# Routing on VectorE in two places: owners behind the state, running counts in front of the masking

## What is computed

```python
def _attn_ref(r, k, v, w, u):
    for t in range(S):
        kt, vt, rt = (k[:, :, t], v[:, :, t], r[:, :, t])
        cur = np.einsum('bhd,bhe->bhde', u[None] * kt, vt)
        y[:, :, t] = np.einsum('bhd,bhde->bhe', rt, state + cur)
        state = w[None, :, :, None] * state + np.einsum('bhd,bhe->bhde', kt, vt)

def _moe_ref(x, w_gate, w1, w2, capacity):
    logits = x @ w_gate
    expert_idx = np.argmax(logits, axis=1)
    ...
    for i in range(N):
        e = expert_idx[i]
        if counts[e] < capacity:
            disp[e, counts[e]] = x[i]
            pos[i] = counts[e]
            counts[e] += 1
            keep[i] = True
    h = np.maximum(np.einsum('ecd,edf->ecf', disp, w1), 0.0)
    y = np.einsum('ecf,efd->ecd', h, w2)
    for i in range(N):
        if keep[i]:
            out[i] = gate_w[i] * y[expert_idx[i], pos[i]]

def _moe2_ref(x, w_in, w_out):
    h = x @ w_in
    g = h - np.tanh(h)
    return (g @ w_out).astype(np.float32)
```

## Time and profile before

| | us |
|---|---|
| median of 3 runs | 419.5 |
| lowest, highest | 415.28, 419.82 |
| the profiled execution | 416.17 |
| its span in the trace | 414.4 |
| TensorE busy in the span | 392.7 |
| VectorE busy | 211.5 |
| ScalarE busy | 182.5 |
| GpSimd busy | 155.2 |

### The profile page before, as it was taken

One profiled execution on the slowest core, in us unless ns is written; L12 is line 12 of the kernel. 1 busy time (PEld: TensorE's weight loads), 2 busy tenths in 40 slices (PEclk: granted clock), 3 DMA queues, 4 the chain that ended last, 5 costly groups with the idle time before them and its releaser, 6 DMA issues.

```text
span 414.4 us, 10465 instructions
## 1 busy us (share of the span) xinstructions
PE 392.7 (95%) x3736; PEld 380.8 (92%) x3737; DVE 211.5 (51%) x453; ACT 182.5 (44%) x486; POOL 155.2 (37%) x132
## 2 busy tenths in 40 slices
PE   5999898999999999999999899999999999999991
PEld 4787777989999999999999899999999999999991
DVE  6365888655556455465455556524343434334340
ACT  5354456432666656657566354533132312231220
POOL 3564676604888815427246043352001100020002
PEclk9999999558999999999999999999999999999997
DMA  7488987443678585685776725101000100010001
GB/s 249 137 253 264 270 247 215 134 153 119 202 241 253 190 269 172 229 262 175 244 232 204 229 69 182 56 1 57 0 0 3 54 0 0 0 57 0 0 1 63
DMA packets 48454, 56.85 MB, mean 137 GB/s; under 512 B 3585, under 2 KB 46017, under 8 KB 48417
## 3 DMA queue, kind: packets, MB, share of 16 engines
q1 hardware_dynamic: 35936, 46.23, 35.5%
q10 hardware_dynamic: 10512, 5.31, 4.5%
q0 software_dynamic: 1968, 4.83, 3.1%
HBM read 46.23 MB, written 10.13 MB: 136 GB/s over the span
## 4 chain that ended last, share of the span: by engine, by line
PE 89%; DVE 5%; issue 2%; DMA 1%; ACT 1%; POOL 0%; POOLq 0%; SPq 0%; DVEq 0%; ACTq 0%
PE ring L1065 13%; PE ring L1067 13%; PE ring L1066 13%; PE pO L1317 8%; PE pO L1316 8%; PE pO L1065 5%; PE pO L1067 5%; PE pO L1066 5%; PE pY L1189 3%; PE pA L1140 2%; PE pD L1094 2%; PE ring L1205 2%; PE pY L1174 1%; PE ring L1254 1%; DVE kw L784 1%
## 5 line engine op out<-in xcount | busy, mean ns | idle before, releaser
L459 POOL TENSOR_TENSOR w_lo<-raw_weights,w_hi 128x768 fp32r<-128x768 f32 x40 | 73.7, 1845 | 85.1 <-ACT w_hi L580 84.9
L1007 DVE SCALAR_TENSOR_TENSOR minus_tanh<-square,ring 128x384 f32<-128x384 f32 x64 | 35.5, 554 | 93.3 <-ACT square L730 93.3
L580 ACT ACTIVATE w_hi<-raw_weights 128x768 fp32r<-128x768 f32 x80 | 67.1, 846 | 24.3 <-DMA raw_weights<-w 24.2
L730 ACT ACTIVATE square<-ring 128x384 f32<-128x384 f32 x64 | 31.5, 491 | 94.3 <-DVE h_hi L1017 53.8
L1065 PE MATMUL ring<-yT_hi,w_hi 128*128 x192 | 65.0, 338 | 1.7 <-DVEq L1002 1.7
L1067 PE MATMUL ring<-yT_hi,w_lo 128*128 x192 | 64.9, 338 | 0.0
L1316 PE MATMUL pO<-w_hi,h_hi 128*128 128x384 f32 x192 | 64.9, 338 | 0.0
L1317 PE MATMUL pO<-w_lo,h_hi 128*128 128x384 f32 x192 | 64.8, 338 | 0.0
L1066 PE MATMUL ring<-yT_lo,w_hi 128*128 x192 | 64.8, 338 | 0.0
L1065 PE MATMUL pO<-h_hi,w_hi 128*128 128x224 f32 x192 | 53.3, 278 | 0.0
L550 POOL DMA_INDIRECT out<-out_rows,tok x12 | 11.7, 974 | 111.1 <-ACT out_rows L725 107.2
(11 more groups left out here) (158 smaller groups left out, 762.3 us busy)
## 6 DMA issues: line engine op xcount, KB each, us to landing
raw_weights<-w SPq DMA_DIRECT2D x80, 384.0 KB, 4.0
x_by_slot<-x ACTq DMA_DIRECT2D x9, 576.0 KB, 5.8
x_expert<-x_by_slot SPq DMA_DIRECT2D x8, 576.0 KB, 5.6
kv<-kv_by_token SPq DMA_DIRECT2D x22, 192.0 KB, 4.3
rkT<-rk_by_feature SPq DMA_DIRECT2D x18, 192.0 KB, 3.8
rkT<-rk_by_feature SPq DMA_DIRECT2D x3, 512.0 KB, 5.3
x_expert<-x_by_slot SPq DMA_DIRECT2D x1, 384.0 KB, 3.0
x_by_slot<-x,sloti POOLq DMA_INDIRECT x12, 4.6
```

The source lines that it names most:

```text
L459: pool.tensor_tensor(lo, unit_raw(2, k), hi.bitcast(F32), ALU.subtract).then_inc(w2_ready, 1)
L580: act.activation(hi, unit_raw(what, k), ACT.Copy).then_inc(w1_hi if what == 1 else w2_hi, 1)
L730: act.activation(sq[:, i % 2, :], ring[i % 4][:, 0:CAP], ACT.Square, scale=THIRD ** 0.5, accum_out=sqsum[:, bass.ds(t * (2 * FC) + i, 1)]) ...
L1007: dve.scalar_tensor_tensor(out=nt[:, i % 2, :], in0=sq[:, i % 2, :], scalar=1.0, in1=ring[i % 4][:, 0:CAP], op0=ALU.subtract, op1=ALU.mult ...
```

## The change

`route1` is cut in two. `owners_of` keeps the steps up to `onehot`; `counts_of` has the `upto` additions, `oh_ready` and `slot_limit`. For groups 0 and 1, `owners_of` stands where `route1` stood, at the end of iterations 5 and 9 (`OWNERS`), and `counts_of` stands in iterations 6 and 10 (`COUNTS`) behind `queries` and in front of the masking. Groups 2 and 3 run both halves one behind the other, as before. The first `low` moves from the end of iteration 10, in front of `route2(1)`, into iteration 11, behind `output(10)` and in front of the last masking. No instruction is added or taken away on any engine, and nothing moves on the others. Of what VectorE waits for, one thing is new: the `x` behind `owners_of` waits for the chain semaphore of `onehot`.

```diff
-ROUTE1 = {5: 0, 9: 1}
+OWNERS = {5: 0, 9: 1}
+COUNTS = {6: 0, 10: 1}
...
-            def route1(g, link):
+            def owners_of(g, link):
...
                 link(dve.tensor_tensor(onehot[:, 0:m], bc(prio[:, :].unsqueeze(1), [P, m, E]),
                                        bc(owners.unsqueeze(2), [P, m, E]), ALU.is_equal))
+
+            def counts_of(g, link):
+
+                first, m = GROUPS[g]
+                owners = allf[:, 0, first:first + m]
                 for i in range(m):
                     link(dve.tensor_tensor(upto[:, first + i + 1, :], upto[:, first + i, :], onehot[:, i, :], ALU.add))
                 dve.sem_inc(oh_ready, 1)
...
                 if n + 1 < STEPS:
                     queries(n + 1)
+                else:
+                    low(0, 0, 0)
+                if n in COUNTS:
+                    counts_of(COUNTS[n], rlink)
                 dve.wait_ge(a_full, n + 1)
...
-                if n == STEPS - 2:
-                    low(0, 0, 0)
                 if n == STEPS - 1:
-                    route1(2, rlink)
+                    owners_of(2, rlink)
+                    counts_of(2, rlink)
                     low(0, 1, 0)
                 if n in ROUTE2:
                     route2(ROUTE2[n], rlink)
-                if n in ROUTE1:
-                    route1(ROUTE1[n], rlink)
+                if n in OWNERS:
+                    owners_of(OWNERS[n], rlink)
...
-            route1(3, rlink)
+            owners_of(3, rlink)
+            counts_of(3, rlink)
```

## The result

The changed kernel took 425.2 us in the median of 4 runs (423.8 to 428.2), the kernel before 417.4 in 4 runs beside it (415.2 to 419.8). The ratio is 1.028, 95% interval 1.022 to 1.035; this ratio and all that follow are taken over undisturbed runs alone and can lie up to 0.9% away from the quotient of the two medians, which is 1.019 here. The profiled execution took 425.6 us, its span is 423.8. A later series of 6 runs gave 1.023 (1.012 to 1.033).

A forecast was written before the change was run, and what follows sets the result against it. TensorE, busy 95% of the span, was taken to bound the kernel. Blocked additions and a low clock would start tile 10's L1189 at 87.3 instead of 73.14, taken as 14 us; 416.2 + 14 = 430 us, range 411 to 434.

The forecast's parts named there:

- its own forecast: Attention stage: delay at the first group and low clock to the stage's end, 430 us, range 427 to 434, chance 0.58.
- only shifted: Stages after attention: their work is not touched by the change, so no term of their own in the sum.
- GpSimd blocks the upto: First group, tile 6: `upto` waits for `vdiag`, `kend` and `rkf` in turn, so `At` comes 2.9 us later.
- What is given back: Behind the first group's `At`, GpSimd being idle: 0.44 us of `kw` and 0.59 of `gsum` saved.
- The clock falls behind this wait: First group: after a TensorE wait of 3 us the clock falls to 0.50 between 51 and 55 us.
- It stays low to the dense matmuls near 95: Tiles 6 to 9 onward: clock stays 0.50, a tile takes 8.57 us against 5.0, 14.2 us in all.
- one of its signs: Tiles 7, 8 and 9: 8.5 us between their L1189s would show the forecast right.
- comes back after one or two tiles: Rival, first group: clock falls but returns, adding 3.6 us a tile, 422 to 425 us; chance 0.06.
- The second group: Tile 10: the 1.33 us wait for `x` goes; if the clock held, `At` 0.8 to 1.5 us later, 0 to 1.3 won.
- The moved w_lo: Before the last masking: 0.95 us hidden by VectorE's 2.61 us wait for TensorE, cost nothing.
- The rival "faster": Attention stage: earlier `x` keeps the clock, dent at 72 us goes, 409 to 412 us; chance 0.18 or 0.19.

The follow-up runs named there:

- e4: Changed kernel, but for groups 0 and 1 `upto` reads a second `onehot` in PSUM and `slot_limit` stands behind `onehot`; 414.4 us against 413.6 before, ratio 1.002.
- e8: Changed kernel, but GpSimd waits for the first group's `oh_ready` in front of `vdiag` of tile 6; 412.7 us against 413.5 for the kernel before, ratio 1.002.
- e1: Kernel before with only the first group split, second group and `w_lo` left as before; 418.3 us against 413.6, ratio 1.013.
- e3: Kernel before with only `w_lo` moved in front of the last masking; 414.5 us against 413.6, ratio 1.003.
- e6: Kernel before with idle TensorE products in the wait for `x` of tile 10 alone; 413.8 us against 413.5, ratio 1.004.
- e10: Changed kernel, GpSimd waiting for both groups' counts and, in tile 10, for `rw` of tile 11 before `rkf`; 418.5 us against 417.2 before, ratio 1.005.
- e2: Kernel before with only the second group split, the rest as before; 414.3 us against 413.6, ratio 1.002.
- e7: Kernel before with idle TensorE products in all waits of the routed tiles and the tail; 412.5 us against 413.5, ratio 1.004.

## Why the prediction was right

It said slower, 430 us in a range of 411 to 434. Measured were 425.2 in the first series: inside the range, but below the 427 to 434 that the prediction gave to its own forecast. Against the profiled execution of before I had added 14 us; the two profiled executions are 9.4 us apart, and the ratio of 1.028 is 11.7 us on 416.2. The direction and the wait behind it came for the reason given. That the size came near has luck in it: the first group cost 2.35 us of waiting and 2.35 of slow clock where the sum had 14, and more than half of the 9.4 us lies in terms that the sum did not have (2.5 in tile 11 and up to the experts, 3.2 in the later stages, of which the prediction said that they are only shifted; 1.5 came back, as this execution was ahead when the group began). Point by point:

- **GpSimd blocks the upto: right, in its pieces.** I had the first three ending with `vdiag`, `kend` and `rkf` and the fourth free; they took 0.72, 0.93, 1.20 and 0.18 us. Predicted for `At` was 2.9 us later; measured from the end of `onehot` it is 4.53 (45.11 to 49.64) against 2.16 (46.64 to 48.80), so 2.4 later. Of the half microsecond too much about 0.2 is GpSimd, which was through with `rkf` 4.06 us behind `onehot` in place of 4.26, as `x` began at once behind `onehot`, without the 0.15 us that I had put there. The other 0.3 lies between the end of `rkf` and `At`, 0.47 us in place of 0.8. e4 and e8 show the cause from both sides. One row that I had called in for it does not bear on instructions with two SBUF inputs: `gsum` of L821 has one, and was held up all the same (0.76 us against 0.17).
- **What is given back: right.** `kw` and `gsum` ran free behind the masking (`gsum` 0.17 us at 51.89 in place of 0.76).
- **The clock falls behind this wait: right in the three traces that show the full wait** (changed kernel twice, e1): TensorE had been idle there for 2.3 to 2.6 us and, after the positions, for another 0.84. Behind shorter waits it held at the first group in the kernel before, e3, e4, e6, e8 and e10 and fell in e2.
- **It stays low to the dense matmuls near 95: wrong, and this is the step that failed.** I had argued from one stretch, 72 to 95 us, in which the tile loop did not bring the clock back. In the changed kernel, twice, and in e1 it was back after a single slow tile. The term was sized at 3.6 us a tile for almost four tiles; the trace has 2.35 us once, and 4.94 us between the L1199s of tiles 7, 8 and 9 where the prediction had 8.5 as one of its signs. What I had called the rival "comes back after one or two tiles", 422 to 425 us with a chance of 0.06, is what the profiled execution did. It was not closed either way: e2 stayed at 0.50 for three tiles, and one run of the changed kernel, 437.3 us at a clock of 0.913, lost more than my forecast. A rule drawn from one execution was treated as fixed where it is a draw in each run.
- **The second group: half wrong.** I expected the wait for `x` to vanish and `At` to come later. `x` did come early. But `rw` took 3.04 us behind an indirect DMA, `rkf` and `vdiag`, and TensorE stopped for another reason that had lain under the wait. e2 puts the whole at 0.2% slower with an interval of 0.2% faster to 0.6% slower; of the 0 to 1.3 us that I had said to be won if the clock held, only the low end fits.
- **The moved w_lo: right**, 0.3% with an interval that includes nothing.
- **The rival "faster"** fell with the second group, and with e6 and e7: even where the mean clock was higher than in the kernel before, the time stayed, though the idle products that raised it may have cost as much.

## What to carry to other kernels

Before small VectorE instructions are moved to where VectorE has time, look at which GpSimd instruction is released just ahead of the new place. A chain of short two-input instructions loses a whole GpSimd instruction per link, and four additions of 0.2 us became 3.2; one input in PSUM, or one wait on GpSimd, takes it away. An instruction with a single SBUF input is not safe by that alone: `gsum` was held up too. A wait that is removed may have covered another at the same matmul: look at other tiles for stops that the profile calls issue. And a loss of TensorE's clock seen in one execution is one draw: compare the mean clock over many runs, on the same chip, before it is given a price.

## What the runs showed that I had not expected

- `rw` waited at 70.85 through three GpSimd instructions in a row, to 73.32, and took 3.04 us (3.05 in the second trace); the `upto` waiting between `vdiag`, `kend` and `rkf` got their turn after each. In both traces the first of the three was the indirect DMA. The 1.82 us of `upto` in the earlier trace rows look alike: it also began beside an indirect DMA and ran to the end of the `rkf` behind it.
- Idle products on TensorE raised the mean clock from 0.970 to 0.982 and won nothing.
- The clock fell to 0.50 behind a wait of 1.72 us in front of the dense layer in the changed kernel, and held behind the same wait in the kernel before.
- The kernel before, unchanged, ran from 406.0 to 422.2 us of span over the three series, with mean clocks of 0.949 to 0.985. The chip matters by itself: the median span was 411.9, 411.7 and 415.5 us on three chips, at the same mean clock of 0.970 or 0.971.
